# Scores of the first batch as unsplit fp32 products of two heads on the two halves of TensorE's rows

## What is computed

```
scores = scale * np.matmul(q, k.transpose(0, 1, 3, 2))
thresh = np.max(scores, axis=-1, keepdims=True) - tau
scores = np.where(scores >= thresh, scores, -1000000000.0)
scores = scores - np.max(scores, axis=-1, keepdims=True)
attn = np.exp(scores)
attn = attn / (np.sum(attn, axis=-1, keepdims=True) + 1e-09)
return np.matmul(attn, v)
```

## Time and profile before

| | |
|---|---|
| median of three runs | 1057.28 us |
| the profiled execution | 1059.02 us |
| its span, first to last instruction | 1057.2 us |
| PE busy | 1012.7 us (96%) |
| DVE busy | 608.7 us (58%) |
| ACT busy | 478.5 us (45%) |
| POOL busy | 414.2 us (39%) |
| first row maximum (tile 0) | starts at 8.42 us |
| row maximum of tile 36 | starts at 100.06 us |

### The profile page before, as it was taken

One profiled execution on the slowest core, in us unless ns is written; L12 is line 12 of the kernel. 1 busy time (PEld: TensorE's weight loads), 2 busy tenths in 40 slices (PEclk: granted clock), 3 DMA queues, 4 the chain that ended last, 5 costly groups with the idle time before them and its releaser, 6 DMA issues.

```text
span 1057.2 us, 19237 instructions
## 1 busy us (share of the span) xinstructions
PE 1012.7 (96%) x7424; PEld 928.2 (88%) x7424; DVE 608.7 (58%) x1211; ACT 478.5 (45%) x1120; POOL 414.2 (39%) x363
## 2 busy tenths in 40 slices
PE   6888899999899998999999999999999999999998
PEld 5667789998799998899988999888888888888998
DVE  6989897568986478786575687443124114114111
ACT  5777776646785646775646653221111121111110
POOL 5769485344765334564413247331211211111000
PEclk9899999999999999899999999999999999999999
DMA  8625212024221033311023137102001000100000
GB/s 246 195 80 172 60 36 60 25 81 127 70 56 46 19 98 110 100 30 37 27 88 111 45 125 275 41 1 72 1 1 40 33 1 37 36 1 3 34 1 35
DMA packets 41275, 70.15 MB, mean 66 GB/s; under 512 B 6624, under 2 KB 22368, under 8 KB 40672
## 3 DMA queue, kind: packets, MB, share of 16 engines
q1 hardware_dynamic: 40880, 68.59, 20.4%
q10 hardware_dynamic: 304, 0.33, 0.1%
HBM read 56.50 MB, written 12.41 MB: 65 GB/s over the span
## 4 chain that ended last, share of the span: by engine, by line
PE 81%; DVE 10%; issue 4%; ACT 3%; POOL 1%; DMA 0%; DVEq 0%; SPq 0%; ACTq 0%; POOLq 0%
PE PB L859 21%; PE PB L860 20%; PE PB L861 20%; PE PB L911 8%; PE PB L886 6%; PE PB L905 5%; DVE probs L1489 4%; DVE neg_s L1478 2%; ACT exps L1216 1%; DVE both_last L1496 1%; DVE mix_v L1544 1%; ACT mix_v L1279 1%; POOL fold_l L777 1%; DMA k_raw<-kT_dram 0%; DVE xT L1537 0%
## 5 line engine op out<-in xcount | busy, mean ns | idle before, releaser
L1754 DVE SCALAR_TENSOR_TENSOR h_lo<-PB,h_hi 128x464 fp32r<-128x464 f32 (+1 forms) x80 | 51.0, 638 | 256.6 <-ACT h_hi L1435 256.6
L1435 ACT ACTIVATE h_hi<-PB 128x464 fp32r<-128x464 f32 (+1 forms) x80 | 44.4, 555 | 329.8 <-PE PB L861 329.8
L1489 DVE SCALAR_TENSOR_TENSOR probs<-neg_s,thresh,exps 128x576 f32<-128x576 f32 x144 | 161.5, 1122 | 0.5 <-PE PB L905 0.3
L1478 DVE TENSOR_SCALAR_CACHE_REDUCE neg_s<-PB,taus 128x576 f32<-128x576 f32 x144 | 117.0, 813 | 35.4 <-PE PB L886 31.9
L1230 ACT ACTIVATE probsT<-PB 128x256 f32<-128x256 f32 (+1 forms) x288 | 102.5, 407 | 52.0 <-PE PB L905 51.4
L861 PE MATMUL PB<-un_h,w1l 128*128 128x464 f32 (+1 forms) x320 | 118.9, 371 | 0.0
L860 PE MATMUL PB<-h_lo,w2h 128*128 128x464 f32 (+1 forms) x320 | 118.8, 371 | 0.0
L859 PE MATMUL PB<-h_hi,w2h 128*128 128x464 f32 (+1 forms) x320 | 118.8, 371 | 0.0
L861 PE MATMUL PB<-h_hi,w2l 128*128 128x464 f32 (+1 forms) x320 | 118.8, 371 | 0.0
L859 PE MATMUL PB<-un_h,w1h 128*128 128x464 f32 (+1 forms) x320 | 118.7, 371 | 0.0
L860 PE MATMUL PB<-un_l,w1h 128*128 128x464 f32 (+1 forms) x320 | 118.5, 370 | 0.0
(11 more groups left out here) (202 smaller groups left out, 2413.5 us busy)
## 6 DMA issues: line engine op xcount, KB each, us to landing
q_raw<-qT_dram SPq DMA_DIRECT2D x62, 160.0 KB, 3.1
k_raw<-kT_dram SPq DMA_DIRECT2D x64, 144.0 KB, 3.1
w_raw<-w_dram SPq DMA_DIRECT2D x8, 1024.0 KB, 8.4
u_scr<-x2T SPq DMA_DIRECT2D x4, 1152.0 KB, 5.0
cd<-cd_scr SPq DMA_DIRECT2D x4, 1032.0 KB, 4.9
v_sb<-v_dram SPq DMA_DIRECT2D x16, 256.0 KB, 2.9
u_in<-u_scr SPq DMA_DIRECT2D x4, 928.0 KB, 5.1
out_dram<-u_in SPq DMA_DIRECT2D x16, 232.0 KB, 2.1
```

The source lines that it names most:

```text
L1478: nc.vector.tensor_scalar(neg_s[:, n % 2, :].rearrange("p (a n) -> p a n", a=2), scores(n), taus[:, 2:3], None, ALU.mult, ALU.min, accum_o ...
L1489: nc.vector.scalar_tensor_tensor(probs[:, n % 2, place_of(n):place_of(n) + S], neg_s[:, n % 2, :], thresh[:, col:col + 1], exps[:, n % 2, ...
L1754: nc.vector.scalar_tensor_tensor(h_lo[:, ft % 3, 0:w], bank(4 + ft % 3)[:, 0:w], 0.0, h_hi[:, ft % 3, 0:w].bitcast(F32), ALU.max, ALU.subt ...
```

## The change

**Scores.** In the first batch the splits are gone. `qk_turn` makes the scores of two tiles at once, the same query rows of both heads: head 0 of the pair lies on partitions 0 to 63 of `q_raw` and `k_raw`, head 1 on 64 to 127, and each product has 64 rows of contraction, plain fp32, 128 query columns. Five products make a turn, in the order head 0 (224 keys), head 1 (288), head 0 (64), head 0 (288), head 1 (288). The two heads write different banks. The mixed tile is two plain fp32 products with all 128 rows (`qk_mixed`). A turn waits until both double banks are read, so `max_ready` >= n where one tile more could be outstanding before.

**Order of tiles.** The heads take turns: places 0, 2, 5, 7 are head 0, places 1, 3, 6, 8 head 1, place 4 stays the mixed tile. VectorE does both row maxima of a turn one behind the other, in the slot of the first, then the two masks. For that there is a third buffer for the negated scores (`neg_third`), and `probs_even`, `probs_odd`, `probs_mixed`, which alternate by turns. ScalarE makes the thresholds of a turn as one instruction of two columns, behind the first exponential. The products with `v_sb` go by turns too, both heads on the two column halves, and so the output of a pair lies in order and is multiplied by one instruction of 128x512 (`turns_out`) in place of four of 64x256.

**Memory and the border to the second batch.** `neg_third`, `probs_odd` and `probs_mixed` lie where the splits lie later. So the split of head 8 (the first of batch two) makes its last step after the mask of tile 32, and that of head 9 begins when all transposes of the first batch are done (`unit_ready` 72), and its steps stand two slots later in GpSimd's order than they did. Loads: a pair of the first batch is loaded whole when all scores of the pair before are made.

The core of the diff:

```diff
+TURNS_FIRST, TURNS_SECOND = (0, 2, 5, 7), (1, 3, 6, 8)
...
+def in_turns(n):
+    return n < TILES_BATCH
+def opens_turn(n):
+    return in_turns(n) and n % TILES_PAIR in TURNS_FIRST
...
+        split = m.put("split", [P128, 2, SQ + 2 * S], F32R)
+        q_hl, k_hi, k_lo = split[:, :, 0:SQ], split[:, :, SQ:SQ + S], split[:, :, SQ + S:SQ + 2 * S]
+        neg_third = Place(at_split + (SQ + S) * 4).put("neg_third", [P128, S], F32)
+        r = Place(at_split + (SQ + 2 * S) * 4)
+        probs_odd = r.put("probs_odd", [P128, 2 * S], F32)
+        probs_mixed = r.put("probs_mixed", [P128, S], F32)
...
                     if step == 1:
-                        pool.wait_ge(qk_in[p], 64 * pair + 64)
-                        if pair > 0:
+                        pool.wait_ge(qk_in[p], 64 * (pair - PAIRS) + 192)
+                        if n == 1:
+                            pool.wait_ge(unit_ready, 2 * TILES_BATCH)
+                        elif n > 1:
                             pool.wait_ge(scores_ready, pair * TILES_PAIR if p else pair * TILES_PAIR - FULL)
...
                 second_head = {0: (1,), 1: (2, 3), 2: (4,)}
+                second_late = {2: (1, 2, 3), 3: (4,)}
...
+                def qk_turn(n):
+                    pair = n // TILES_PAIR
+                    if n % TILES_PAIR == 0:
+                        pe.wait_ge(qk_in[pair % 2], 64 * (pair // 2) + 64)
+                    if n >= 2:
+                        pe.wait_ge(max_ready, n)
...
+                    def part(h, half, at, keys):
+                        partitions = slice(h * DH, (h + 1) * DH)
+                        width = keys.stop - keys.start
+                        return nc.tensor.matmul(scores(n + h)[:, half, at:at + width], q_raw[partitions, pair % 2, rows], k_raw[partitions, pair % 2, keys],
+                                                start=True, stop=True)
+                    part(0, 0, DH, slice(0, HALF - DH))
+                    part(1, 0, 0, slice(0, HALF))
+                    part(0, 0, 0, slice(S - DH, S))
+                    part(0, 1, 0, slice(HALF - DH, S - DH)).then_inc(scores_ready, 1)
+                    part(1, 1, 0, slice(HALF, S)).then_inc(scores_ready, 1)
+                def qk_mixed(n):
+                    pair = n // TILES_PAIR
+                    pe.wait_ge(max_ready, n - 1)
+                    for half in range(2):
+                        last = nc.tensor.matmul(scores(n)[:, half, :], q_raw[:, pair % 2, FULL * P128:SQ], k_raw[:, pair % 2, half * HALF:(half + 1) * HALF],
+                                                start=True, stop=True)
+                    last.then_inc(scores_ready, 1)
...
+                    if in_turns(n):
+                        place = slice(row_of(n) * P128, (row_of(n) + 1) * P128)
+                        for kt in range(KT):
+                            weights = [v_sb[:, kt, pair % 2, head * DH:(head + 1) * DH] for head in range(2)]
+                            moving = [probsT[:, block_of(n if kt == KT - 1 else t, kt), :] for t in (n - 1, n)]
+                            last = both_halves(outputs(pair)[:, place], (weights[0], moving[0]), (weights[1], moving[1]),
+                                               jj == 1 and kt == 0, jj == TILES_PAIR - 1 and kt == KT - 1)
...
+                def threshold(n, tiles):
+                    act.wait_ge(max_ready, n + tiles)
+                    col = n % (2 * TILES_PAIR)
+                    nc.scalar.activation(thresh[:, col:col + tiles], negmax[:, col:col + tiles], ACT.Identity, bias=taus[:, 1:2]).then_inc(thr_ready, tiles)
...
+                def turns_out(pair):
+                    dve.wait_ge(pv_ready, (pair + 1) * PAIR_GROUPS)
+                    dve.wait_ge(inv_copied, pair * 2 + 2)
+                    nc.vector.tensor_tensor(out_tile(pair)[:, 0:FULL * P128], outputs(pair), inv_rows[:, DH:], ALU.mult).then_inc(x_out, 4)
...
+                    at_once = opens_turn(n) and n + 2 < TILES_BATCH
+                    if n < TILES and not (n and opens_turn(n - 1) and n + 1 < TILES_BATCH):
                         row_max(n)
+                    if at_once:
+                        row_max(n + 1)
                     if 0 <= n - 1 < TILES:
                         mask(n - 1)
```

184 lines of the change are left out of this document (117 added, 67 removed).

## The result

The changed kernel takes 1049.89 us (median of four runs, 1049.28 to 1050.52). The kernel before, run beside it, takes 1056.76. The ratio is 0.9935, with a 95% interval of 0.9917 to 0.9952. The forecast was 1049.3. The profiled execution took 1050.13 us, its span is 1048.1 (1057.2 before). The traces differ by 9.1 us and the medians by 6.9, because the profiled execution before was 2.3 us above the median of its four runs (1059.02) and the changed one 0.2. Which stretch of the old trace holds this scatter, the runs do not tell, so differences between the two traces may be too large by some 2 us in all.

The account below looks back on a forecast made before the run. VectorE was taken to bound pairs 1 to 3, its masks held back by GpSimd. Gains of 8.8 (three pairs) and 0.2 (pair 0) less 1.0 (border) give 8.0 us: 1057.28 to 1049.3 us; 8-in-10 range 1038 to 1060.5.

Parts of the forecast that it names:

- The three pairs: Pairs 1 to 3 of the first batch: 21.0 us a pair, 63.0 against 71.8, a gain of 8.8 us.
- VectorE's work: VectorE's undisturbed work per first-batch pair: 16.6 us before, 15.5 after, with one output of 0.7 us replacing four.
- The contention that stays: VectorE's masks and `both_last` slowed by GpSimd's two-operand SBUF operations: 2.6 of 5.1 us a pair stay, bounds 1.5 and 5.1.
- How much of the contention adds: Of 2.6 us a pair VectorE still loses to GpSimd, 1.5 lengthens the pair; the rest lies under waits.
- The turn: TensorE's five score products for two tiles: row halves partly overlap, 1.25 us, bounds 0.96 and 1.91, plus 0.3 for shape changes.
- changes of tile shape: TensorE switching tile shapes: 0.15 us a change, so 0.3 us more a turn, bounds 0 and 0.6.
- The handovers: VectorE's waits for TensorE's next scores at five places a pair: 0.9, 0.3, 0.1, 2.1, 0.6, together 4.0 us.
- Pair 0: Program start: first turn 2.5 us plus 0.3, as at half clock; row maximum 0 at 9.5 us; gain 0.2 us.
- The border: Passage to batch two: head 9's split ready 1.5 us late, cost taken as 1.0 us, bounds 0 and 2.5; load hidden.
- (B): Rival: VectorE alone paces, row halves overlap fully (0.96 us), shape changes are free: 1041.2 us, chance 20%.
- (C): Rival: TensorE's row halves do not overlap, a turn takes 1.91 us, the kernel gets slower: 1061.1 us, chance 14%.
- (D): Rival: GpSimd still slows VectorE's masks, 5.1 us a pair stay and 4.1 add: 1057.1 us, no change, chance 16%.

Follow-up runs that it names:

- The weights' run: Changed kernel with GpSimd's first-batch subtractions for gate, key weights and both tables replaced by zero fills, low parts left out: 1047.97 us.
- the contention put back: Changed kernel with GpSimd given back, on scratch memory, the four split operations per head for heads 1 to 7 in the first batch: 1053.24 us.
- The run with the heads in sequence: Changed kernel with a turn's five products ordered head 0 three times, then head 1 twice: 1055.27 us.
- the two runs that moved one: Changed kernel with mixed-tile scores one slot earlier, 1050.02 us; or with mixed output products and spreads of pairs 0 to 2 behind the next pair's first turn, 1050.73 us.
- the warm start: Changed kernel with eleven 512-column products of zeros on TensorE ahead of its first work: 1049.06 us.
- The runs with a faster first batch: Changed kernel with mixed scores and the exponential before them earlier, 1051.41 us; those plus eleven zero products and heads alternating throughout a turn, 1048.81 us.

## Why the prediction was right, point by point

**The bound.** Right. VectorE set the pace through the masks: taking GpSimd's subtractions out of the old order gives 6.8 us, putting them into the new one costs 3.4. The gain was forecast at 8.0 us and is 6.9 by the medians.

**The three pairs.** Forecast 63.0 us, measured 63.2. The account of a pair: 15.5 us of VectorE's own work, its waits, and what GpSimd takes. In the trace the waits of pairs 1 to 3 are 15.8 less the 2.6 before the first row maximum and the 4.2 of pair 0, which is 9.0, or 3.0 a pair. The contention is 6.9, all of it in these three pairs, as GpSimd is idle in pair 0: 2.3 a pair in the mean (4.8, 1.1 and 1.1). 15.5 + 3.0 + 2.3 = 20.8, with 21.1 measured; waits before masks (0.7 in all) are the rest. The forecast had 15.5 + 4.0 + 1.5 = 21.0.

**VectorE's work.** The prediction's terms for the kernel before add up to 16.3 us (13.4 + 0.35 + 0.8 + 1.75), not 16.6, and so to 15.2 for the changed one, not 15.5. The trace leaves 15.5, so there is 0.3 us of work in it that was not listed. The one output takes 0.68 (0.7 forecast). The contention that stays was put at 2.6 a pair. It is 2.3 in pairs 1 to 3, but 1.7 over all four, since none is left in pair 0: 6.9 us of 20.5, a third and not half. The masks have a mean of 0.984 where 1.04 was named.

**How much of the contention adds.** The step that was mis-sized: 1.5 of 2.6, or 58%. The weights' run gives 33% to 45%, the contention put back 23% to 30%. If these shares hold for what is left, the undisturbed waits must be longer than the 4.0 forecast, 3.0 plus what the contention fills, about 1.3 to 1.8, so 4.3 to 4.8. The two errors have opposite signs, and the sum hid them: that the three pairs came out at 63.2 for 63.0 is in this part luck.

**The turn.** 1.28 us, for a stream put at 1.25. The starts within a turn spread over 1.0 us, as forecast. The run with the heads in sequence bears out the model: 1.65 for 1.67. The 0.3 us for changes of tile shape were too much: 0.03 is what the measured turn has above the stream model, and the model itself misses the other two orders by -0.02 and 0.07. The page "TensorEngine Tiling (Array Packing)" of the Trainium skill (Key Properties) says that TensorE drains at such a switch. No run here isolates a switch, and if there is a drain it costs hardly anything beside these pieces.

**The handovers.** The wait before the mixed row maximum is 1.6 us in pairs 1 to 3, not 0.9. Before a pair's first row maximum VectorE waits 2.03, 0.55 and 1.51 us, where 2.1 was forecast for each: 1.36 in the mean, and with 0.55 the largest miss of the five. It was named as the longest wait of a pair and is that at the first border only; at the other two the 1.62 before the mixed tile is longer. Two of the five were also rounded up by 0.1 in the prediction (1.65 less 1.44 is 0.2, 5.0 less 3.0 is 2.0), so its terms give 3.8, not 4.0. That a wait removed would come back elsewhere was not forecast, and the two runs that moved one show it.

**Pair 0.** First turn 2.50 us (2.5 forecast), row maximum 0 at 9.28 (9.5), gain 0.65 (0.2). That the start is slow for want of work on TensorE ahead of it is shown by the warm start, and that it is the lower clock level by durations, as said there.

**The border.** One wait for `split` at the mixed tile of pair 4, 2.37 us, as named. It cost 0.4 us of the head start, not 1.0. The load of head 9 was called hidden, and it is, but barely: its last part is issued at 90.14 us and lands about 5.1 later, 0.3 us before GpSimd's split starts at 95.53. The runs with a faster first batch have no such margin.

**The rivals.** (B) did not come: a turn is longer than full overlap, 0.96, would make it. (C) is excluded by the heads in sequence, whose 1055.3 us is also far below the 1061.1 at which C was priced. (D) had the wrong price: with nearly all the contention back the time is 1053.2, not 1057.1, since D let 4.1 of 5.1 us a pair add. 

**The rest.** As it was: in the traces 8.9 us are gained at tile 40 and 9.1 at the end. TensorE is busy 87%, 90% and 92% in pairs 1 to 3, where over 90% was named.

## What to carry to other kernels

When an engine is slowed by another one's use of memory, what it costs is not the time lost but the part that no wait covers: 78% to 85% in an order where the slowed engine sets the pace, 23% to 45% in one where it alternates with TensorE. So measure it in the order that will be run, and expect two remedies for one bound to overlap (6.8 and 4.5 us alone, 7 together). When a wait is taken away and the time stays, look in the trace for where it came back, and look beyond the stretch as well: here a pair 0 that stayed slow for longer and a queue of stores ahead of one load had eaten the gain, and to put the load ahead of these five stores gave 2.2 us back at the border.

## What was not expected of the hardware

TensorE starts the program at about half speed (turns that last 2.50 us instead of 1.35), though the profile's windows show no low grant in that stretch. Eleven products of zeros ahead of the work bring it to full speed from the first turn on. It can be lost again: in one of the three kernels that have them the second turn took 2.32 us, in a window with a granted clock of 0.52. Waits of TensorE of 3.7 us and windows with TensorE busy 56% are followed here by stretches at the low grant, so a wait can cost more than its length: the eight products behind it took 2.24 us for 1.32. And how far plain fp32 products on the two halves of the rows overlap depends on the order in which they stand: the same five products take 1.22, 1.28 or 1.65 us.
